# An attention, token-mixing and gating chain on one core: 512-token blocks, quarter-array attention, queries turned by VectorE, no filler matmuls

## Chip, cores and metric

The kernel runs on one core of a Trainium2 chip. The metric is the device time of one execution in microseconds; lower is better.

## What is computed

Three stages follow one another on 8 batches of 576 tokens and 512 channels. All data are 32-bit floats.

```
attn:  8 heads of 64 channels; inside chunks of 64 tokens:
       softmax(q k^T / 8) v                       -> x   (8, 576, 512)
moe:   h = relu(x^T w_tok1) w_tok2                (576 -> 256 -> 576, over tokens)
       u = x + h^T
       x2 = u + relu(u w_ch1) w_ch2               (512 -> 1536 -> 512, over channels)
moe2:  h = relu(x2 w_in); u, v = halves of h      (512 -> 2 x 512)
       v_n = layer norm of v;  v_s = w_spatial v_n + b_spatial   (over tokens)
       out = (u * v_s) w_out
```

Products with weights are made in two parts. A value is split into a high part (its fp32r rounding) and a low part (the rest), and three fp32r matmuls (high x high, high x low, low x high) add up. ScalarE makes the high part while it empties the accumulator, and VectorE makes the low part.

## The kernel before

The program is written engine by engine, with every wait given by hand as a semaphore count. The first phase makes attention and the channel mixing up to x2, batch after batch, and stores x2 in DRAM; the second phase (lines L1053 and after for TensorE) reads x2 in pairs of batches and makes the gating unit. TensorE's first phase is a list of slots.

**Channel mixing.** Each batch's 576 tokens are cut into a half of 256 and a half of 320 (`SPLIT`). For each half, 12 groups of 128 hidden channels are made by `up` (12 matmuls, L1188, into one of two `hid_bank`) and consumed by `down` (12 matmuls, L1206, into four `acc_bank`). A batch has 24 slots; slot s runs `up` of group s+2, then the side jobs of table `SIDE`, then `down` of group s. ScalarE (`hidden`, L649) and VectorE (L832) turn a finished `hid_bank` into `hidh` and `hidl`.

**Side jobs.** Between them stand the jobs that prepare the next batch: for each of its five tiles of 128 tokens (the fifth has 64) `TQ` (queries transposed by TensorE, L1106), `SC` (scores, L1115), `PT` (the probabilities transposed, L1122) and `PV` (values, L1131); then `M` (token mixing up, L1144 to L1149), and `U0`, `U1` (token mixing down plus x, L1071 to L1082) for the two halves. In `SC` a full 128x128 stationary operand with zeroed off-diagonal parts takes two heads at once. A 32-bit matmul of `SC` or `PV` appears in the trace as two instructions. Keys are turned by VectorE from the second batch on (`turn`, L788): SyncE loads them as 32-column blocks (`load_blocks`, L418, 16 DMAs of 16 KB per tile), and VectorE transposes 32x32 blocks. Queries and values come in one DMA per tile (L404).

**Order.** SyncE issues all loads and stores in program order, on one queue. `next_tiles` gives its order of the loads of the next batch. The batches 0 to 6 of the first phase are a hardware loop on every engine, as is the second phase; batch 7 is written out. The prologue (`PRO`, `PRO_ACT`, `PRO_DVE`) makes batch 0's attention and token mixing; `WARM` puts filler matmuls of the identity (L1225) ahead of some of its jobs. GpSimd clears operands, scales the probabilities in the prologue, and makes the low parts of the weights.

Of the kernel before, what the change touches and what calls it, by code (L numbers as in the profile page):

```python
# [30 lines left out]
def build(nc, q, k, v, w_tok1, w_tok2, w_ch1, w_ch2, w_in, w_spatial, b_spatial, w_out, out, x2_dram):
# [24 lines left out]
    SCALE = 1.0 / float(D) ** 0.5

    def rows(t):
        return P if t < KS else REM

    SLOTS = 2 * KF
    SIDE = {0: [("U1", 0), ("U1", 1)], 1: [("U1", 2), ("U1", 3)], 2: [("TQ", 0)], 3: [("SC", 0)], 4: [("TQ", 1)],
# [6 lines left out]

    TURN = {2: 0, 4: 1, 7: 2, 10: 3, 13: 4}

    LAST_SIDE = {0: SIDE[0], 1: SIDE[1]}
    for n in range(NT):
        LAST_SIDE[10 + n] = [("WT", n)]
    LAST_SIDE[10 + NT] = [("WR", 0), ("WR", 1)]  # L80

    def jobs(text):
        return [(kind, int(t)) for kind, t in (x.split(".") for x in text.split())]

    PRO = jobs("TQ.0 TK.0 TQ.1 TK.1 SC.0 TQ.2 TK.2 SC.1 PT.0 TQ.3 TK.3 SC.2 PV.0 PT.1 TQ.4 TK.4 SC.3 PV.1 PT.2 "
               "SC.4 PV.2 PT.3 PT.4 PV.3 PV.4 M.0 M.1 U0.0 U0.1 U0.2 U0.3")


    PRO_ACT = jobs("TQ.0 TK.0 TQ.1 TK.1 EX.0 TQ.2 TK.2 EX.1 PT.0 TQ.3 TK.3 EX.2 PV.0 PT.1 TQ.4 TK.4 EX.3 PV.1 PT.2 "
                   "TW.0 TW.1 EX.4 PV.2 PT.3 PT.4 TW.2 PV.3 PV.4 CW.0 CW.1 M.0 CW.2 M.1 CW.3 U0.0 U0.1 U0.2 U0.3")
    PRO_DVE = jobs("SH.0 NO.0 SH.1 NO.1 SH.2 NO.2 PV.0 SH.3 NO.3 PV.1 SH.4 NO.4 PV.2 PV.3 PV.4 "
                   "M.0 M.1 U0.0 U0.1 U0.2 U0.3")
# [1224 lines left out]
```

## Time and profile before

| | us |
|---|---|
| time, median of 3 runs | 1360.36 (1359.75 to 1360.47) |
| the profiled execution, its own time | 1359.22 |
| its span in the profile | 1357.4 |
| TensorE busy | 1343.2 (99%) |
| VectorE busy | 528.3 (39%) |
| ScalarE busy | 418.6 (31%) |
| GpSimd busy | 64.2 (5%) |
| DMA queue of SyncE, share of 16 engines | 20.2% |

Busy time counts each engine's instructions, overlaps once. The trace models the ends of pipelined matmuls, so durations of single matmuls overlap; the distance from start to start is what one costs in a stream. Issuing DMAs is not counted as busy, but the timeline shows each issue on SyncE with its duration.

### The profile page before, as it was taken

How to read it: one execution, taken by the hardware profiler on the slowest of the kernel's cores; microseconds unless marked ns; L12 is line 12 of the kernel's file. 1: busy time of each engine (PE TensorE's matmuls, PEld its weight loads, DVE VectorE, ACT ScalarE, POOL GpSimd, SP SyncE). 2: the span in 40 equal slices, each digit the busy share in tenths (PEclk: the TensorE clock that was granted, in tenths of full speed). 3: DMA queues.
4: the chain of work that ended last, by engine and by line, in shares of the span. 5: the costliest groups of instructions: out<-in, count | busy, mean ns of one | idle time of the engine just before them, and what ended most of it. 6: DMA issues, size and time to landing. Idle time of an engine off the chain costs nothing.

```text
span 1357.4 us, 26091 instructions
## 1 busy us (share of the span) xinstructions
PE 1343.2 (99%) x9485; PEld 1291.7 (95%) x9485; DVE 528.3 (39%) x1167; ACT 418.6 (31%) x843; POOL 64.2 (5%) x45
## 2 busy tenths in 40 slices
PE   9999999999999999999999999999999999999998
PEld 9999999999999999999999999999998998998997
DVE  3343234234224324423432342234563463463461
ACT  6532133123213312321321331123433433433332
POOL 3800000000000000000000000122000000000000
PEclk9999999999999999999999999999999999999999
DMA  9523021212302211220230210312021021021002
GB/s 251 127 53 67 21 42 42 40 38 40 66 22 44 54 26 43 55 45 25 53 67 21 42 34 1 130 47 90 1 87 55 0 76 63 0 70 70 1 1 70
DMA packets 183429, 70.57 MB, mean 52 GB/s; under 512 B 159184, under 2 KB 171088, under 8 KB 183312
## 3 DMA queue, kind: packets, MB, share of 16 engines
q1 hardware_dynamic: 183312, 68.98, 20.2%
q8 instruction: 78, 1.28, 0.4%
q14 instruction: 39, 0.32, 0.1%
HBM read 50.05 MB, written 18.87 MB: 51 GB/s over the span
## 4 chain that ended last, share of the span: by engine, by line
PE 99%; issue 1%; ACT 0%; POOL 0%; POOLq 0%
PE bank L1053 31%; PE bank L1206 23%; PE bank L1188 23%; PE bank L1131 5%; PE bank L1115 5%; PE bank L1071 4%; PE bank L1144 3%; PE bank L1106 1%; PE bank L1079 1%; PE bank L1122 1%; PE bank L1225 1%; PE bank L1149 0%; PE bank L1148 0%; PE bank L1082 0%; PE bank L1165 0%
## 5 line engine op out<-in xcount | busy, mean ns | idle before, releaser
L832 DVE SCALAR_TENSOR_TENSOR hidl<-bank,hidh 128x256 fp32r<-128x256 f32 (+1 forms) x192 | 88.0, 458 | 438.6 <-ACT hidh L649 438.6
L1206 PE MATMUL bank<-hidh,w2h 128*128 128x256 f32 (+1 forms) x768 | 237.1, 309 | 0.0
L1188 PE MATMUL bank<-uh,w1h 128*128 128x256 f32 (+1 forms) x768 | 228.3, 297 | 7.8 <-issue 7.8
L1188 PE MATMUL bank<-uh,w1l 128*128 128x256 f32 (+1 forms) x768 | 227.3, 296 | 0.0
L1188 PE MATMUL bank<-ul,w1h 128*128 128x256 f32 (+1 forms) x768 | 227.3, 296 | 0.0
L1206 PE MATMUL bank<-hidh,w2l 128*128 128x256 f32 (+1 forms) x768 | 227.1, 296 | 0.0
L1206 PE MATMUL bank<-hidl,w2h 128*128 128x256 f32 (+1 forms) x768 | 226.7, 295 | 0.0
L649 ACT ACTIVATE hidh<-bank 128x256 fp32r<-128x256 f32 (+1 forms) x192 | 78.9, 411 | 456.6 <-PE bank L1188 456.6
L1188 PEld LDWEIGHTS bank<-uh,w1h 128*128 128x128 f32 x768 | 145.8, 190 | 9.9 <-issue 9.3
L1206 PEld LDWEIGHTS bank<-hidh,w2h 128*128 128x128 f32 x768 | 145.4, 189 | 1.6
L1206 PEld LDWEIGHTS bank<-hidl,w2h 128*128 128x128 f32 x768 | 145.6, 190 | 0.5
L1188 PEld LDWEIGHTS bank<-ul,w1h 128*128 128x128 f32 x768 | 145.8, 190 | 0.0
L1188 PEld LDWEIGHTS bank<-uh,w1l 128*128 128x128 f32 x768 | 145.7, 190 | 0.0
L1206 PEld LDWEIGHTS bank<-hidh,w2l 128*128 128x128 f32 x768 | 145.2, 189 | 0.0
L1053 PE MATMUL bank<-wsh,nl 128*128 128x256 f32 (+1 forms) x256 | 75.8, 296 | 0.0
L1053 PE MATMUL bank<-wsl,nh 128*128 128x256 f32 (+1 forms) x256 | 75.7, 296 | 0.0
L1053 PE MATMUL bank<-wsh,nh 128*128 128x256 f32 (+1 forms) x256 | 75.7, 296 | 0.0
L1115 PE MATMUL bank<-k_t,q_t 128*128 128x64 f32 x576 | 68.8, 271 | 0.0
L1115 PEld LDWEIGHTS bank<-k_t,q_t 128*128 128x128 f32 x576 | 67.5, 192 | 0.1
L1053 PE MATMUL bank<-x2h,winl 128*128 128x384 f32 x192 | 64.2, 334 | 0.0
L1053 PE MATMUL bank<-x2h,winh 128*128 128x384 f32 x192 | 64.2, 334 | 0.0
L1053 PE MATMUL bank<-x2l,winh 128*128 128x384 f32 x192 | 64.2, 334 | 0.0
(158 smaller groups left out, 2356.7 us busy)
## 6 DMA issues: line engine op xcount, KB each, us to landing
x2l_raw<-x_scratch SPq DMA_DIRECT2D x32, 256.0 KB, 4.3
out<-out_tile SPq DMA_DIRECT2D x32, 256.0 KB, 2.0
qn<-in_q SPq DMA_DIRECT2D x30, 256.0 KB, 3.2
vn<-in_v SPq DMA_DIRECT2D x30, 256.0 KB, 3.9
kn<-in_k SPq DMA_DIRECT2D x448, 16.0 KB, 1.7
x_scratch<-x_half SPq DMA_DIRECT2D x8, 640.0 KB, 4.2
x_scratch<-x_half SPq DMA_DIRECT2D x8, 512.0 KB, 3.3
w1l_raw<-in_moe_w_ch SPq DMA_DIRECT2D x6, 512.0 KB, 9.1
```

Of the source, the lines that this page charges most:

```text
L649: nc.scalar.activation(hidh[:, g % 3, 0:n], hid_bank[g % 2][:, 0:n], ACT.Relu).then_inc(hid_hi, 1)
L832: return nc.vector.scalar_tensor_tensor(lo, src, 0.0, hi.bitcast(F32), op0=ALU.max, op1=ALU.subtract)
L1053: last = nc.tensor.matmul(dst, w, x, start=(n == 0), stop=(n == len(operands) - 1))
L1071: last = nc.tensor.matmul(bank[:, 0:width(h)], w, x, start=(m == 0 and e == 0), stop=(m == KT - 1 and e == 2))
L1079: nc.tensor.matmul(dst, x[:, s, cs], ident_r[:, :], is_transpose=True, start=False, stop=False)
L1106: last = nc.tensor.transpose(bank[:, g * P:g * P + n], src[:, g * P:(g + 1) * P], ident[0:n, 0:n])
L1115: last = nc.tensor.matmul(bank[:, c0:c0 + CHUNK], q_t[:, t % 2, g, a, :], k_t[:, t % 2, g, a * CHUNK:(a + 1) * CHUNK], start=True, stop=True)
L1122: last = nc.tensor.transpose(bank[0:n, g * P:(g + 1) * P], prob[:, t % 2, g, 0:n // CHUNK, :].rearrange("p a k -> p (a k)"), ident[:, :])
L1131: last = nc.tensor.matmul(bank[0:n, h * D:(h + 1) * D], p_buf(i, t)[0:n, h, 0:n], nat_tile(i, "v", t)[:, h, :], start=True, stop=True)
L1144: nc.tensor.matmul(bank[:, :], w, x, start=(e == 0), stop=False)
L1188: last = nc.tensor.matmul(hid_bank[g % 2][:, 0:width(h)], w, x, start=(c == 0 and e == 0), stop=(c == KC - 1 and e == 2))
L1206: last = nc.tensor.matmul(acc_bank[c][:, 0:n], w, x, start=(f == 0 and e == 0), stop=(f == KF - 1 and e == len(ops) - 1))
```

## The change

The first phase is written anew. The second phase keeps its computation.

- **Blocks.** The 4608 tokens of all batches are cut into 9 blocks of 512 for the channel mixing, in place of 16 halves. Block j takes the first 512-64j tokens of batch j (`UA`) behind the last 64j tokens of batch j-1 (`UB`). `up` and `down` run as `up 0, up 1, down 0, up 2, down 1, ...` (`GROUPS`), with side jobs behind single groups (`PLAN`, `REST`, `SPATIAL`). Where a boundary cuts a 128-token tile, x is added by ordinary matmuls with 64 columns of the identity.
- **Quarters.** `SC` and `PV` use 64x64 operands at the four quarters of the array: 16 matmuls of 64x64 by 64 per tile each, results in two banks.
- **Queries.** From batch 1 on `TQ` is gone. SyncE loads queries as blocks, as it does keys (16 more DMAs per tile, in place of one), and VectorE turns both (`turn`). Values come in four DMAs per tile (two for the 64-row tile).
- **Loads.** `qn`, `kn` and `vn` hold two tiles each. The next load of q and k waits until VectorE has turned the tile two before; the next load of v waits for the `PV` two before. The order is the loop `for j in range(B - 1)` below. In the prologue the first loads of batch 1 stand between the channel weights.
- **Waits and hand-overs.** `q_t`, `k_t` are single buffers; `ul` is added on GpSimd (`add_low`); x2 takes the place of `uh` and is stored in eight DMAs per block.
- **Prologue.** `WARM` is empty, `M` starts in parts (`MP`) as tiles of x are ready, VectorE scales the probabilities, two groups of channel weights (`CW_EARLY`) are rounded ahead in place of four, and the others follow `hidden` of block 0 on ScalarE.
- **Loops.** All hardware loops are written out.

```diff
--- before.py
+++ after.py
+    BW = 512
+    NB = B * S // BW
+    assert NB * BW == B * S and NB == B + 1 and S - BW == REM
...
+    def share(kind, b):
+        cut = BW - REM * b
+        return (0, cut, b, REM * b) if kind == "UA" else (cut, S, b + 1, 0)
...
+    GROUPS = [("up", 0), ("up", 1)]
+    for f in range(KF):
+        GROUPS += [("down", f)] + ([("up", f + 2)] if f + 2 < KF else [])
+    NG = len(GROUPS)
+    PLAN = {2: "SC.0", 5: "SC.1", 6: "PT.0", 7: "PV.0", 8: "SC.2", 9: "PT.1", 10: "PV.1", 11: "SC.3", 12: "PT.2",
+            13: "PV.2", 14: "SC.4", 15: "PT.3", 16: "PV.3", 17: "PT.4", 18: "PV.4", 19: "M.0", 20: "M.1",
+            21: "UA.0 UA.1", 22: "UA.2 UA.3"}
+    REST = {3: "UB.0 UB.1", 4: "UB.2 UB.3"}
+    SPATIAL = {9: "WT.0", 10: "WT.1", 11: "WT.2", 12: "WT.3", 13: "WT.4", 14: "WR.0", 15: "WR.1"}
+    def behind(j, g):
+        if j > B - 1:
+            return []
+        side = jobs(j, REST.get(g, ""))
+        if j < B - 1:
+            return side + jobs(j + 1, PLAN.get(g, ""))
+        return side + jobs(0, SPATIAL.get(g, ""))
+    PRO_PE = jobs(0, "TQ.0 TK.0 TQ.1 TK.1 SC.0 TQ.2 TK.2 SC.1 PT.0 TQ.3 TK.3 PV.0 SC.2 PT.1 TQ.4 TK.4 PV.1 SC.3 PT.2 "
+                     "PV.2 SC.4 PT.3 MP.0 PV.3 PT.4 MP.1 PV.4 MP.2 MP.3 M.0 M.1 UA.0 UA.1 UA.2 UA.3")
+    PRO = [job for job in PRO_PE if job[0] != "MP"]
+    PRO_ACT = jobs(0, "TQ.0 TK.0 TQ.1 TK.1 EX.0 TQ.2 TK.2 EX.1 PT.0 TQ.3 TK.3 EX.2 PV.0 PT.1 TQ.4 TK.4 EX.3 PV.1 PT.2 "
+                      "TW.0 TW.1 EX.4 PV.2 PT.3 TW.2 PV.3 PT.4 CW.0 PV.4 CW.1 M.0 M.1 UA.0 UA.1 UA.2 UA.3")
+    PRO_DVE = jobs(0, "SH.0 NO.0 SH.1 NO.1 SH.2 NO.2 PV.0 SH.3 NO.3 PV.1 SH.4 NO.4 PV.2 PV.3 PV.4 "
+                      "M.0 M.1 UA.0 UA.1 UA.2 UA.3")
...
-    WARM = {("TQ", 0): 9, ("TQ", 1): 6, ("TQ", 2): 8, ("PV", 2): 7, ("PT", 4): 2}
+    WARM = {}
...
+            def load_v(b, t):
+                for h2 in range(2):
+                    for a in range(rows(t) // CHUNK):
+                        s0 = t * P + a * CHUNK
+                        src = v_in[b, :, s0:s0 + CHUNK, :].rearrange("(g e) s d -> e s g d", e=2)
+                        sp.dma_start(v_tile(b, t)[h2 * CHUNK:(h2 + 1) * CHUNK, :, a, :],
+                                     src[h2, :, :, :]).then_inc((v_loaded if b > 0 else v_first)[t], DMA)
+            def load_blocks(buf, src, b, t, loaded):
                 for h2 in range(2):
                     for e in range(D // BLK):
                         p0 = h2 * D + e * BLK
-                        dst = k_blocks(t)[p0:p0 + BLK, :].rearrange("p (g j e) -> p g j e", g=PAIRS, e=BLK)
+                        dst = blocks(buf, b, t)[p0:p0 + BLK, :].rearrange("p (g j e) -> p g j e", g=PAIRS, e=BLK)
                         for g in range(PAIRS):
-                            src = k[b, 2 * g + h2, t * P:t * P + rows(t), e * BLK:(e + 1) * BLK]
+                            part = src[b, 2 * g + h2, t * P:t * P + rows(t), e * BLK:(e + 1) * BLK]
                             sp.dma_start(dst[:, g, :, :],
-                                         src.rearrange("(j r) e -> r j e", r=BLK)).then_inc(k_loaded[t], DMA)
-            for t in range(NT + 2):
+                                         part.rearrange("(j r) e -> r j e", r=BLK)).then_inc(loaded[t], DMA)
+            def load_qk(b, t):
+                n = later(b, t)
+                if n >= 2:
+                    sp.wait_ge(q_t_ready, NT + n - 1)
+                    sp.wait_ge(k_t_ready, NT + n - 1)
+                load_blocks(qn, q_in, b, t, q_loaded)
+                load_blocks(kn, k_in, b, t, k_loaded)
+            def load_v_next(b, t):
+                n = later(b, t)
+                if n >= 2:
+                    sp.wait_ge(side_full, number["PV", 1 + (n - 2) // NT, (n - 2) % NT])
+                load_v(b, t)
+            for t in range(NT + 1):
                 if t < NT:
...
+                if g == 1:
+                    load_qk(1, 0)
+                if g == 2:
+                    load_v_next(1, 0)
+                    load_qk(1, 1)
+                if g == 3:
+                    load_v_next(1, 1)
...
+            for j in range(B - 1):
+                b = j + 1
+                if j > 0:
+                    store_x2(j - 1)
+                more = b + 1 < B
+                load_qk(b, 3)
+                load_qk(b, 4)
+                load_v_next(b, 2)
+                if more:
+                    load_qk(b + 1, 0)
+                load_v_next(b, 3)
+                if more:
+                    load_qk(b + 1, 1)
+                load_v_next(b, 4)
+                if more:
+                    load_qk(b + 1, 2)
+                    load_v_next(b + 1, 0)
+                    load_v_next(b + 1, 1)
...
+            def add_low(j):
+                for c in range(KC):
+                    pool.wait_ge(acc_free, KC * j + c + 1)
+                    nc.gpsimd.tensor_tensor(x2[j % 2][:, c, :], x2[j % 2][:, c, :], ul[j % 2][:, c, :].bitcast(F32),
+                                            ALU.add).then_inc(x2_ready, 1)
...
+                        if j == 0 and f < NCW - CW_EARLY:
+                            channel_high(CW_EARLY + f)
...
+            def turn(b, t):
+                n = tile_no(b, t)
+                loads = b * (4 * PAIRS * DMA)
+                before = (b, t - 1) if t > 0 else (b - 1, KS)
+                dve.wait_ge(side_full, number[("SC",) + before])
+                for buf, dst, loaded, ready in ((qn, q_t, q_loaded, q_t_ready), (kn, k_t, k_loaded, k_t_ready)):
+                    dve.wait_ge(loaded[t], loads)
+                    nc.vector.transpose(dst[:, :, 0:rows(t)].bitcast(U32),
+                                        blocks(buf, b, t).bitcast(U32).rearrange("p (g s) -> p g s", g=PAIRS)
+                                        ).then_inc(ready, 1)
...
+                    two, qt, kt = both(job), q_tile(b, t), k_tile(b, t)
                     for g in range(PAIRS):
-                        for a in range(2 if t < KS else 1):
-                            c0 = (2 * g + a) * CHUNK
-                            last = nc.tensor.matmul(bank[:, c0:c0 + CHUNK], q_t[:, t % 2, g, a, :],
-                                                    k_t[:, t % 2, g, a * CHUNK:(a + 1) * CHUNK], start=True, stop=True)
+                        for e in range(2):
+                            for a in range(n // CHUNK):
+                                r, s = slice(e * D, (e + 1) * D), slice(a * CHUNK, (a + 1) * CHUNK)
+                                last = nc.tensor.matmul(two[s, e, g * CHUNK:(g + 1) * CHUNK], qt[r, g, s], kt[r, g, s],
+                                                        start=True, stop=True)
...
+                    two, pt, vt = both(job), p_tile(b, t), v_tile(b, t)
+                    for g in range(PAIRS):
+                        for e in range(2):
+                            for a in range(n // CHUNK):
+                                r, s = slice(e * CHUNK, (e + 1) * CHUNK), slice(a * CHUNK, (a + 1) * CHUNK)
+                                last = nc.tensor.matmul(two[s, e, 256 + g * D:256 + (g + 1) * D], pt[r, g, s],
+                                                        vt[r, g, a, :], start=True, stop=True)
...
+            for job in PRO_PE:
+                kind, _, t = job
+                for _ in range(WARM.get((kind, t), 0)):
+                    nc.tensor.matmul(hid[:, 1, 0:P], ident[:, :], ident[:, :], start=True, stop=True)
+                if kind == "MP":
+                    pe.wait_ge(part_lo, parts["PV", 0, t])
+                    if t == 0:
+                        pe.wait_ge(wlo, 2)
+                    for m in range(KT):
+                        token_up(m, hid[:, m, :], t)
+                else:
+                    side_job(job)
+
```

## Rows read from the trace of the kernel before

**Rows 1.** The page, its part 4: shares of the chain that ended last.

```profile
PE 99%; issue 1%; ACT 0%; POOL 0%; POOLq 0%
```

**Rows 2.** Windows by stage: prologue, five whole batches, second phase (columns in first line).

```profile
core 0: us, PE busy (x) PEld busy (x) DVE busy (x) ACT busy (x) POOL busy (x), PEclk, DMA share, GB/s
0.00:45.74 45.74, 43.26 (x344) 41.05 (x345) 16.39 (x33) 32.55 (x54) 24.28 (x22) 1.00 1.01 250
...
164.33:741.27 576.94, 570.27 (x4400) 560.27 (x4401) 209.32 (x421) 153.45 (x315) 0.00 (x0) 1.00 0.20 43
...
937.81:1357.40 419.59, 415.65 (x2336) 381.44 (x2336) 195.13 (x497) 148.75 (x302) 0.00 (x0) 1.00 0.13 43
```

**Rows 3.** Waits of TensorE: in total, times, longest.

```profile
PE bank L1188 <- issue: 7.8, 6, 1.5
```

**Rows 4.** Timeline of SyncE: start, us, k blocks of the last batch, 16 issues each.

```profile
755.67 7.47 SPq L418 DMA_DIRECT2D kn<-in_k  x16
...
765.40 8.30 SPq L418 DMA_DIRECT2D kn<-in_k  x16
...
776.71 8.63 SPq L418 DMA_DIRECT2D kn<-in_k  x16
```

**Rows 5.** The page, its part 6: KB each, median us to landing.

```profile
vn<-in_v SPq DMA_DIRECT2D x30, 256.0 KB, 3.9
kn<-in_k SPq DMA_DIRECT2D x448, 16.0 KB, 1.7
```

**Rows 6.** Timeline of TensorE: first and last of 512, 256 and 320 column runs.

```profile
35.65 0.39 PE L1144 MATMUL bank<-xh,t1h 128*128 128x512 f32 x1
...
37.47 0.39 PE L1144 MATMUL bank<-xh,t1l 128*128 128x512 f32 x1
...
53.74 0.28 PE L1206 MATMUL bank<-hidh,w2h 128*128 128x256 f32 x1
...
54.70 0.28 PE L1206 MATMUL bank<-hidh,w2l 128*128 128x256 f32 x1
...
699.75 0.31 PE L1188 MATMUL bank<-uh,w1h 128*128 128x320 f32 x1
...
701.37 0.31 PE L1188 MATMUL bank<-uh,w1l 128*128 128x320 f32 x1
```

**Rows 7.** Timeline of TensorE: a TQ, a PV of 64 rows, an SC, with neighbours.

```profile
61.86 0.60 PE L1106 MATMUL bank<-ident,qn 128*128 128x128 f32 x4
...
62.22 0.36 PE L1206 MATMUL bank<-hidh,w2h 128*128 128x256 f32 x1
...
128.68 0.31 PE L1188 MATMUL bank<-uh,w1l 128*128 128x320 f32 x1
128.92 1.14 PE L1131 MATMUL bank<-vn,p_t 64*64 64x64 f32 x16
...
130.24 0.31 PE L1206 MATMUL bank<-hidl,w2h 128*128 128x320 f32 x1
...
650.23 1.90 PE L1115 MATMUL bank<-k_t,q_t 128*128 128x64 f32 x16
651.93 0.36 PE L1206 MATMUL bank<-hidh,w2h 128*128 128x256 f32 x1
```

**Rows 8.** Groups by line and form, VectorE: busy us, mean ns, idle before.

```profile
L801 DVE TENSOR_REDUCE smax<-bank 128x8 f32<-128x512 f32 x32 | 22.1, 692 | 45.9 <-PE bank L1115 45.8
...
L788 DVE STREAM_TRANSPOSE k_t<-kn 128x512 uint32<-128x512 uint32 x28 | 19.7, 702 | 0.0
```

**Rows 9.** Timeline of SyncE in the prologue.

```profile
17.18 0.77 SPq L427 DMA_DIRECT2D t1l_raw<-in_moe_w_tok  x1
...
19.82 0.47 SPq L434 DMA_DIRECT2D w1l_raw<-in_moe_w_ch  x1
```

**Rows 10.** Timeline of TensorE: the first and the fourth group of filler matmuls.

```profile
1.53 3.94 PE L1225 MATMUL bank<-ident 128*128 128x128 f32 x18 [1.53 <-POOL ident L539]
...
26.15 1.78 PE L1225 MATMUL bank<-ident 128*128 128x128 f32 x14
```

More of the change, by code:

```diff
@@ L103, in listing @@
-    def listing(table):
-        return [j for s in range(SLOTS) for j in table.get(s, [])]
-    BODY, LAST = listing(SIDE), listing(LAST_SIDE)
-    PRO_BANKS = 6
-    def order(i):
-        return PRO if i is None else (LAST if isinstance(i, int) and i == B - 1 else BODY)
-    def bank_of(i, idx):
-        return idx % (PRO_BANKS if i is None else 2)
-    def number(i, job):
-        return order(i).index(job) + 1
-    def parts(i, job):
-        seq = order(i)
-        return sum(j[0] in TWO_PART for j in seq[:seq.index(job) + 1])
@@ L129, in build, with tile_no @@
+    number = {job: n + 1 for n, job in enumerate(SEQ)}
+    parts = {}
+    for job in SEQ:
+        if job[0] in TWO_PART:
+            parts[job] = len(parts) + 1
+    in_bank = {n: [job for job in SEQ if n in BANKS[job]] for n in range(8)}
+    def tile_no(b, t):
+        return b * NT + t
     with ExitStack() as ctx:
@@ L277, in build @@
         side_full = sem("side_full")
-        side_free = [sem(f"side_free{b}") for b in range(PRO_BANKS)]
         q_t_ready = sem("q_t_ready")
@@ L518, in store_out @@
                                      out_tile[bb * REM:(bb + 1) * REM, n % 2, :]).then_inc(s, DMA)
-            def pair(j, last):
-                if not last:
+            for j in range(NP):
+                if j < NP - 1:
                     sp.wait_ge(full, j * NJ + job_no(("U", NU - 1)))
@@ L567, in _ @@
                 split(c, winh[:, c, :], winl_raw[:, c, :], winl[:, c, :])
+            add_low(B - 1)
+            add_low(NB - 1)
             pool.wait_ge(wout_loaded, DMA)
+            for c in range(KC):
+                pool.wait_ge(x2_stored[c], stored(NB - 1))
             for c in range(KC):
@@ new lines, in _ @@
+            for j in range(NB):
+                if j > 0:
+                    residual(j - 1)
+                for g, (kind, f) in enumerate(GROUPS):
+                    if kind == "up":
+                        hidden(j, f)
+                    if j == 0 and g == 1:
+                        turn(1, 0)
+                    for job in behind(j, g - 1) if g > 0 else []:
+                        if job[0] == "SC":
+                            softmax_norm(job[1], job[2])
+                    for job in behind(j, g):
+                        if job[0] == "SC":
+                            softmax_shift(job[1], job[2])
+                            n = later(job[1], job[2]) + 1
+                            if n < (B - 1) * NT:
+                                turn(1 + n // NT, n % NT)
+                        elif job[0] in TWO_PART:
+                            side_job(job)
@@ L937, in stats @@
+            for piece in range(KC):
+                split_x2(0, piece)
+            residual(NB - 1)
+            for b in range(4, 8):
+                dve.sem_inc(free[b], 1)
+            for piece in range(KC, X2_PIECES):
+                split_x2(0, piece)
             def stats(j, n):
@@ L1008, in gate_low @@
                 r.then_inc(g_lo, 1)
-            def pair(j, last):
-                gates = [m for kind, m in PHASE2 if kind == "SP"]
+            dve.wait_ge(bias_loaded, DMA)
+            for j in range(NP):
                 for n in range(NJ):
@@ L1085, in side, with token_up @@
[L1085 to L1104 removed]
+            def token_up(t, bank, s):
+                cols = slice(t * P, (t + 1) * P)
+                for e, (w, x) in enumerate(three(t1h[:, s, cols], t1l[:, s, cols], xh[:, s, :], xl[:, s, :])):
+                    nc.tensor.matmul(bank, w, x, start=(s == 0 and e == 0), stop=False)
```

828 lines of the change are left out of this document (353 added, 475 removed), and 6 rows, old and new, of the table SIDE.

## The prediction

> **What bounds the kernel now.** I read the page first: the chain that ended last is TensorE for 99% [rows 1]. TensorE's waits come next: 7.8 us in six stops of up to 1.5 us, released by no engine; they stand where the batch loop turns [rows 3]. So before, time is the sum of TensorE's instructions. The windows cut it: 45.74 us of prologue, 576.94 us for five batches (115.4 each), 419.59 us of second phase [rows 2], which the change leaves alone. Then the queue that the change loads most: SyncE, where the k blocks of the batch written out without a loop show what one DMA issue costs [rows 4].
>
> **TensorE, part by part.** Pitches from start to start: 512 columns (37.47 - 35.65)/8 = 0.227 us; 256 columns 0.96/8 = 0.120; 320 columns 1.62/11 = 0.147 [rows 6]. Each is the columns at 2.4 GHz plus 0.013.
> - `up` and `down`: before 8 x 24 x 12 = 2304 matmuls at 0.120 and as many at 0.147, 615 us. After 9 x 24 x 12 = 2592 at 0.227, 588 us. Gain 27.
> - Loop turns gone: gain 8 [rows 3].
> - `TQ` gone in 7 batches: a job costs 0.36 us plus 0.08 on the next matmul [rows 7], so some 0.44 x 28 plus 7 of the short tile, 15 us.
> - `SC` and `PV` in quarters. A full-array `SC` takes 1.70 us for 16 instructions, 0.107 each. The only quarter jobs in the trace are the `PV` of the 64-row tile: 16 instructions, and from 128.68 to 130.24 they cost 1.56 - 2 x 0.147 = 1.27 us; 1.14 busy less a matmul's tail is about 0.93, or 0.058 each, and 0.34 is for going into and out of that shape [rows 7]. After, a tile has 32 such instructions. One at a time: 32 x 0.058 + 0.34 = 2.2 us. Four at a time: 0.46 + 0.34 = 0.8. No row shows two quarters side by side. I take 1.5, the middle, since 2.2 is the nearest row but all its instructions used the same quarter. Over 56 jobs that is a gain of 56 x (1.78 - 1.5) = 16 (1.78: the 1.70 and 0.08 on the next matmul), between a loss of 24 and a gain of 55.
> - Token mixing: same columns; 32 extra matmuls where tiles are cut and a few narrow ones: loss 4, bounds 2 and 6.
>
> The row says that a lone 64-row job pays 0.34 us for its shape and that its instructions follow at 0.058. The Trainium skill (TensorEngine Tiling (Array Packing), Key Properties) has a rule for each side: changing the tiling mode drains the engine, and different tiles execute weight loads and matmuls in parallel. By the first alone the 56 jobs would lose 24 us; with both they would gain 55.
>
> TensorE's own work after the prologue would then be: 588 + 84 (56 x 1.5) + 15 (14 short `SC` and `PV` at 1.1) + 16 (`PT`) + 45 (`M`, 14 jobs of 14 matmuls at 0.227) + 74 (token mixing) + 3 (the spatial transposes) = 825 us, against 892 (937.81 - 45.74) before.
>
> **VectorE, ScalarE, GpSimd.** A turn costs VectorE 0.70 us, twice per tile now, in place of once [rows 8]; per block about 5 x 0.7 us more on an engine 39% busy. ScalarE loses the two `TQ` copies. GpSimd gets `add_low`, free after the prologue. I cost these at nothing as long as `turn` finds its data; but `turn` waits for a DMA inside VectorE's queue, and behind it stand the low parts that `down` waits for.
>
> **SyncE: the new chain.** Before, a tile took 16 DMAs for k, one for q, one for v. After, 32 for q and k, and 4 for v: 178 per batch in place of 90. Three straight runs of 16 took 7.47, 8.30 and 8.63 us [rows 4], so one issue costs 24.4/48 = 0.508 us (0.467 to 0.539). It is the queue's pace, not the transfer: a block lands 1.7 us after issue [rows 5]. A tile's q and k need 32 x 0.508 = 16.3 us, while `SC` jobs stand three groups apart: 3 x 12 x 0.227 = 8.2 us plus some 2 of side jobs. Only two tiles of buffer stand between.
>
> Follow block j (1 to 5), from its start. `SC.0` stands behind group 2: 8.2 + 1.7; then the two VectorE passes over the scores and the two turns of tile 1, 4 x 0.7 = 2.8, and 0.3 for semaphores: 13.0. Only now may SyncE load tile 3. Its order up to the values of tile 4 is q,k 3; q,k 4; v 2; q,k 0 of the next batch; v 3; q,k 1 of the next batch; v 4. That is 128 + 10 = 138 issues x 0.508 = 70.1, plus 2 to land: 85.1. TensorE would want `PV.4` at about 74 (19 groups x 2.72 = 51.7 plus the side jobs before it, 22), so it stops some 11 us. Behind `PV.4` (1.3) come five groups (13.6), `M` (6.4) and `UA` (4.0 on average): 25.3. A block takes 110.4 us, whatever the quarters cost; five take 552.
>
> Block 0 is later still, since SyncE comes to it from the prologue. The first channel weight was issued at 19.82 [rows 9]; 13 more v issues push it to between 20 and 26, I take 23. From there to the last value of tile 4 of batch 1 stand 12 weight DMAs, 7 tiles of q and k (224) and 18 of v: 254 x 0.508 = 129.0. So 23 + 129 + 2 = 154, and with the tail (`PV.4` 1.3, groups 13.6, `M` 6.4, `UA` of 448 columns 6.4) block 0 ends at 181.7. The prologue itself hides: its first `up` I put at 49 (45.74 plus 3 for the 256 columns that move into it), and its missing fillers cost nothing on this chain. ScalarE's wait for the fourth weight group inside block 0 hides behind it too.
>
> Block 6 has no next loads in front of its values and is TensorE's own: 65.4 + 12 + 2.2 + 2.3 + 6.4 + 9 = 97. Block 7 is 65.4 + 8.5 + 3 = 77, block 8 is 65.4.
>
> **Sum.** 181.7 + 552 + 97 + 77 + 65.4 = 973.1; 1 for the hand-over; 419.6 for the second phase: span 1393.7.
>
> The stops also cost clock. Each stretch of the trace reads a granted clock of 1.00 [rows 2], yet the first group of fillers, after 1.53 us of idle, took 3.94/18 = 0.219 us per instruction and a later one 1.78/14 = 0.127 [rows 10]: the 1.2 GHz level against the 2.4 GHz level, 18 x 0.092 = 1.7 us lost. Six stops at `PV.4` of some 10 us: 10.2 (bounds 0 and 15). Span 1404; 1.8 around it (1359.22 against 1357.4) and 1.1 up to the median (1360.36 against 1359.22): **1407 us**.
>
> The bounds: at 0.467 per issue the chain's 254 + 690 issues take 39 less, and without clock loss 10 less: 1358. At 0.539 they take 29 more, and the prologue 3: 1439. Quarters at 2.2 add about 11 (`SC.0` and `PV.4` in six blocks, all jobs in block 6).
>
> **Rivals.**
> - *SyncE keeps up (faster).* Mechanism: the issue pace in straight code is set by something that the new program doesn't have, and each q,k tile is there when `turn` asks. For it: SyncE needs only 186 issues per block, stores among them, 94 of 110 us, so it isn't full, only badly placed; DMA engines are 20% busy. Against it: 0.47 stands between nearly all issues of the three runs. Then TensorE's sum holds: 49 + 825 + 419.6 + 3 + 3 = 1300 us (quarters between: 1258 to 1341). It decides below about 0.46 us per issue: the chain must lose 47 us over 944 issues, 0.05 each, for the forecast to meet 1360.
> - *Half of it.* The chain exists, but stops hide in block slack, and gains and stops cancel: about 1360.
> - *Code fetch and queue.* All code is straight now. The runs of rows 4 differ by single slow issues (7.47 against 8.63 for the same 16). If such gaps grow with the doubled list, one issue costs 0.56 and the chain gives 1407 + 944 x 0.052 = 1456.
> - *Quarters one at a time*: 1418, within the forecast's range.
>
> The Trainium skill (DMA: Bandwidth & Descriptors, Anatomy of one DMA, written for the other descriptor path) gives about 50 ns for the dispatch of a DMA and says that many descriptors can be emitted before their cost shows. By that price the 944 issues would take 47 us and the first rival would hold; the rows of SyncE show ten times as much, and the measurement decides.
>
> **Chances.** Forecast (1358 to 1439): 0.60. SyncE keeps up: 0.31. Half: 0.04. Code fetch: 0.05. So faster by over 0.2%: 0.32; within 0.2%, about what a measurement of this kernel can tell from no change: 0.04; slower: 0.64. The range reaches down to 1295, which leaves out about four tenths of the first rival, and up to 1440: together 0.2 left out. The forecast's own range is 1358 to 1439.
>
> **What would show it.** In the profile after: SyncE's q and k issues back to back for most of a block, 16 in about 8 us; TensorE idle ahead of `PV` of the last tile, released by a DMA of v, some 10 us in each of blocks 0 to 5, and in block 0 stops ahead of several jobs; first phase's blocks of 110 us, then 97, 77 and 65. VectorE's turns with idle time released by DMA of q. `up` and `down` at 0.227. The quarters show as distances within `SC` and `PV`: 0.058 is one at a time. The prediction is wrong if issues of q and k come faster than 0.46 us, if TensorE has no stops, or if the second phase is longer than 420 us.

## The result

The changed kernel takes 1416.05 us (median of 4 runs, 1415.86 to 1417.48) against 1360.15 for the one before: a ratio of 1.0413, 95% interval [1.0395, 1.0431]. It is slower by 56 us. The profiled execution's span is 1414.0 us.

The page of the changed kernel, its parts 1, 2 and 4. TensorE is busy for fewer microseconds than before (1289.0 in place of 1343.2), and the chain that ended last, all TensorE before [rows 1], is now SyncE's queue for a quarter:

```profile
PE 1289.0 (91%) x8385; PEld 1091.8 (77%) x8385; DVE 527.7 (37%) x1079; ACT 335.7 (24%) x647; POOL 102.2 (7%) x73
...
PEclk8897799799889889979979999999999999999999
...
PE 69%; SPq 26%; issue 3%; DMA 1%; DVE 0%; ACT 0%
SPq L459 22%; PE hid L1147 15%; PE acc L1162 14%; PE acc L1027 13%; PE hid L1027 8%; PE side L1027 8%; SPq L449 3%; PE side L1036 3%; PE side L1062 2%; PE side L1048 2%; DMA vn<-in_v 1%; PE side L1055 1%; PE side L1105 1%; PE side L1089 1%; SPq L441 1%
```

L459 issues the blocks of q and k, L449 the values. `up` is L1147, `down` L1162, `SC` L1089, `PT` L1094, `PV` L1105. The waits of TensorE (us in total, times, longest) name above all one transfer; the stops of [rows 3] are gone:

```profile
PE side L1105 <- DMA vn<-in_v: 97.2, 14, 9.1
PE side L1078 <- DMA q_pro<-in_q: 5.3, 2, 4.3
PE acc L1078 <- DVE xl L832: 3.9, 1, 3.9
```

Windows of the changed kernel, cut at the first `up` (57.44), at the starts of blocks 1 and 6 (192.20, 757.70) and at the end of block 8 (994.53), with the columns of [rows 2]:

```profile
0.00:57.44 57.44, 40.56 (x432) 31.42 (x433) 22.17 (x40) 24.26 (x41) 15.74 (x13) 0.82 0.64 157
57.44:192.20 134.76, 107.38 (x710) 86.46 (x708) 42.62 (x73) 27.76 (x46) 19.90 (x9) 0.85 0.28 59
192.20:757.70 565.50, 488.69 (x3542) 397.75 (x3540) 197.61 (x356) 99.18 (x185) 25.54 (x21) 0.91 0.21 42
757.70:994.53 236.83, 236.83 (x1371) 194.76 (x1369) 69.87 (x119) 45.02 (x83) 28.48 (x21) 1.00 0.17 50
994.53:1414.00 419.47, 415.55 (x2337) 381.38 (x2335) 195.48 (x494) 139.45 (x293) 12.55 (x12) 1.00 0.13 43
```

Where SyncE has loads of the next batch ahead of its values (blocks 0 to 5), TensorE idles and its granted clock is below 1. Blocks 6 to 8 and the second phase have no idle time beyond the usual, and the clock is 1.00. The second phase is that of before (419.59). So the whole loss stands in the prologue and in blocks 0 to 5.

SyncE's timeline in block 2 (306.16 to 421.51): start, time over which the issues run, count.

```profile
317.87 9.06 SPq L459 DMA_DIRECT2D qn<-in_q  x16
326.98 7.55 SPq L459 DMA_DIRECT2D kn<-in_k  x16
334.62 8.24 SPq L459 DMA_DIRECT2D qn<-in_q  x16
...
363.27 7.67 SPq L459 DMA_DIRECT2D kn<-in_k  x16
370.99 2.58 SPq L449 DMA_DIRECT2D vn<-in_v  x4
373.66 7.66 SPq L459 DMA_DIRECT2D qn<-in_q  x16
381.37 7.55 SPq L459 DMA_DIRECT2D kn<-in_k  x16
388.96 1.26 SPq L449 DMA_DIRECT2D vn<-in_v  x2
```

And TensorE's in the same block, its two long stops and what follows the first (a third stop, of 1.4 us, stands ahead of `PV.2`):

```profile
375.87 1.13 PE L1105 MATMUL side<-vn,p_t 64*64 64x64 f32 x32 [9.09 <-DMA vn<-in_v]
376.93 0.79 PE L1147 MATMUL hid<-uh_a,w1h 128*128 128x512 f32 x1
...
377.94 0.63 PE L1147 MATMUL hid<-uh_a,w1l 128*128 128x512 f32 x1
378.37 0.63 PE L1147 MATMUL hid<-uh_a,w1h 128*128 128x512 f32 x1
...
392.18 1.12 PE L1105 MATMUL side<-vn,p_t 64*64 64x64 f32 x16 [6.85 <-DMA vn<-in_v]
```

From 317.87 to 390.22 SyncE issues without a break (the three rows left out are of the same kinds). The four value DMAs of tile 3 end at 373.57 and land 2.3 us later: there `PV.3` starts. The two of tile 4 end at 390.22 and land 2.0 us later: there `PV.4` starts. Behind the stop a 512-column matmul takes 0.43 us (378.37 - 377.94) in place of 0.227.

### The profile page after: what moved, and what is told of

Same layout as the page of the kernel before. It is cut to its first block, busy times and chain, and to the rows that moved or that the text cites. A ratio compares the mean times of both kernels' runs of the same rounds, so it can differ in the third digit from the quotient of the medians.

```text
span 1414.0 us, 20802 instructions
## 1 busy us (share of the span) xinstructions
PE 1289.0 (91%) x8385; PEld 1091.8 (77%) x8385; DVE 527.7 (37%) x1079; ACT 335.7 (24%) x647; POOL 102.2 (7%) x73
## 2 busy tenths in 40 slices
DMA packets 226495, 70.35 MB, mean 50 GB/s; under 512 B 203296, under 2 KB 213152, under 8 KB 226400
## 3 DMA queue, kind: packets, MB, share of 16 engines
q1 hardware_dynamic: 226400, 69.02, 20.0%
## 4 chain that ended last, share of the span: by engine, by line
PE 69%; SPq 26%; issue 3%; DMA 1%; DVE 0%; ACT 0%
SPq L459 22%; PE hid L1147 15%; PE acc L1162 14%; PE acc L1027 13%; PE hid L1027 8%; PE side L1027 8%; SPq L449 3%; PE side L1036 3%; PE side L1062 2%; PE side L1048 2%; DMA vn<-in_v 1%; PE side L1055 1%; PE side L1105 1%; PE side L1089 1%; SPq L441 1%
## 5 line engine op out<-in xcount | busy, mean ns | idle before, releaser
L1162 PE MATMUL acc<-hidh,w2h 128*128 128x512 f32 x432 | 176.5, 409 | 0.0
L1162 PE MATMUL acc<-hidl,w2h 128*128 128x512 f32 x432 | 170.3, 394 | 0.0
L1162 PE MATMUL acc<-hidh,w2l 128*128 128x512 f32 x432 | 170.2, 394 | 0.0
L1105 PE MATMUL side<-vn,p_t 64*64 64x64 f32 x1008 | 29.9, 254 | 97.2 <-DMA vn<-in_v 97.2
L1105 PEld LDWEIGHTS side<-vn,p_t 64*64 64x64 f32 x1008 | 24.9, 161 | 110.1 <-issue 110.1
L1147 PE MATMUL hid<-uh_a,w1h 128*128 128x512 f32 x240 | 103.6, 432 | 0.0
L1147 PE MATMUL hid<-ul_a,w1h 128*128 128x512 f32 x240 | 99.4, 414 | 0.0
L1147 PE MATMUL hid<-uh_a,w1l 128*128 128x512 f32 x240 | 98.7, 411 | 0.0
L1162 PEld LDWEIGHTS acc<-hidh,w2l 128*128 128x128 f32 x432 | 82.1, 190 | 18.2
L1162 PEld LDWEIGHTS acc<-hidh,w2h 128*128 128x128 f32 x432 | 82.1, 190 | 17.6
L1162 PEld LDWEIGHTS acc<-hidl,w2h 128*128 128x128 f32 x432 | 82.3, 190 | 15.1
L1147 PE MATMUL hid<-uh_b,w1h 128*128 128x512 f32 x192 | 82.8, 431 | 0.0
L1147 PE MATMUL hid<-ul_b,w1h 128*128 128x512 f32 x192 | 79.3, 413 | 0.0
L1147 PE MATMUL hid<-uh_b,w1l 128*128 128x512 f32 x192 | 78.8, 410 | 0.0
L1147 PEld LDWEIGHTS hid<-uh_a,w1h 128*128 128x128 f32 x240 | 48.7, 203 | 11.4
L1147 PEld LDWEIGHTS hid<-uh_a,w1l 128*128 128x128 f32 x240 | 48.5, 202 | 11.2
L665 ACT ACTIVATE prob<-prob 128x512 f32<-128x512 f32 (+1 forms) x40 | 25.3, 632 | 130.6 <-DVE prob L815 130.6
L1147 PEld LDWEIGHTS hid<-ul_a,w1h 128*128 128x128 f32 x240 | 48.9, 204 | 9.4
```

The costliest lines, as they stand in the source:

```text
L1105: last = nc.tensor.matmul(two[s, e, 256 + g * D:256 + (g + 1) * D], pt[r, g, s], vt[r, g, a, :], start=True, stop=True)
L1147: last = nc.tensor.matmul(hid[:, n % 2, :], w, x, start=(c == 0 and e == 0), stop=(c == KC - 1 and e == 2))
L1162: last = nc.tensor.matmul(acc[:, c, :], w, x, start=(f == 0 and e == 0), stop=(f == KF - 1 and e == len(ops) - 1))
```

## The experiments

Times are medians, ratios are to the kernel before as run beside each. The main theory: SyncE issues a DMA every 0.5 us, the loads of q, k stand ahead of the values in one queue, and their number sets the length of a block. The rivals were the quarters, the filler matmuls, and the turning of queries as such.

### Queries in one DMA per tile

```diff
-                load_blocks(qn, q_in, b, t, q_loaded)
+                sp.dma_start(qn[0:rows(t), n % 2, :].rearrange("p (h d) -> p h d", h=H),
+                             q_in[b, :, t * P:t * P + rows(t), :].rearrange("h s d -> s h d")).then_inc(q_loaded[t], DMA)
...
```

> The changed kernel, but from batch 1 on a tile's queries come in one DMA in place of 16, in their natural layout, and VectorE turns that; what is left out is the right layout of q, so scores of batches 1 to 7 are of other numbers, while every instruction on TensorE, VectorE and ScalarE stays. SyncE issues 103 DMAs per batch in place of 178. Theory (the issues of SyncE set the blocks): the 97 us of TensorE stops ahead of PV go, and the first phase falls to TensorE's own sum, 57 (prologue) + 795 + 419.5 = 1272 us of span, 1275 measured. Rival (the stops come from something else, such as the values' four DMAs, code written out without loops, or VectorE's second transpose): above 1380.

1278.77 us, ratio 0.9406 [0.9387, 0.9425], span 1276.7, near the theory's 1275. No wait for values is left; the largest of TensorE's are now those of the prologue:

```profile
PE side L1079 <- DMA q_pro<-in_q: 5.4, 3, 4.2
PE acc L1106 <- DVE xl L833: 4.9, 2, 3.7
```

Blocks 1 to 5 run from 156.62 to 620.38, TensorE busy in every microsecond:

```profile
156.62:620.38 463.76, 463.76 (x3541) 378.84 (x3540) 197.06 (x356) 99.19 (x185) 25.54 (x21) 1.00 0.23 51
```

This run gives the split of the loss. For the same instructions the changed kernel took 565.50 us: 76.8 of idle time and 488.69 - 463.76 = 24.9 of slower matmuls. The idle time is ten stops of 6.7 to 9.1 us and the one of 1.4, so that a long stop is 7.5 us of waiting and some 2.5 us of slow clock. Fifteen issues fewer per tile bring 137 us in all. The bytes are the same (the same tile in one piece). The packets fall too, from 226,400 to 185,744 on this queue, but the 16 engines were busy for 20.0% with them and are for 21.0% without, and a block of 16 KB landed 1.8 us after its issue. So what costs is the number of issues, not the transfers.

### The value loads on another queue

ScalarE issues the values of the tile two later once it has emptied a `PV`; SyncE keeps all loads of q and k.

```diff
-                if n >= 2:
-                    sp.wait_ge(side_full, number["PV", 1 + (n - 2) // NT, (n - 2) % NT])
-                load_v(b, t)
+                if n < 2:
+                    load_v(b, t)
...
+                    m = later(b, t) + 2
+                    if b > 0 and m < (B - 1) * NT:
...
+                                act.dma_start(v_tile(vb, vt)[h2 * CHUNK:(h2 + 1) * CHUNK, :, a, :],
+                                              src[h2, :, :, :]).then_inc(v_loaded[vt], DMA)
```

> The changed kernel, but the values of batches 1 to 7 (from their third tile) are issued by ScalarE right after it has emptied the PV of two tiles before, in place of SyncE behind 64 to 128 issues of q and k. Same DMAs, same data, other queue. Theory: the values no longer stand behind q and k, the stops ahead of PV go; what is left is the pace of q and k, seen as VectorE waiting in turn for k of the next batch: blocks 1 to 5 of 97 to 101 us in place of 113, total about 1330 (1310 to 1350). Rival (issue pace is shared by all queues, or the transfer itself is slow): 1390 or more.

1329.28 us, ratio 0.9777 [0.9758, 0.9797], as the theory had it (1330). The wait for values is gone; what is late next is one step up the same queue. Waits of TensorE, and of VectorE for a DMA:

```profile
PE side L1102 <- DVE xl L840: 23.5, 6, 5.3
...
DVE k_t L811 <- DMA kn<-in_k: 67.2, 12, 8.8
```

VectorE stands in `turn`, waiting for k, with the low part of x queued behind (L840), and TensorE's next `PT` (L1102) waits for the bank that VectorE has yet to read. So 87 us of the changed kernel's loss come from the values standing behind q and k on one queue (118 value issues have also left SyncE), and some 50 stay with the number of q and k DMAs (1329 against 1279).

### Values ahead of the next batch's q and k, same queue

```diff
                 load_v_next(b, 2)
-                if more:
-                    load_qk(b + 1, 0)
                 load_v_next(b, 3)
                 if more:
-                    load_qk(b + 1, 1)
+                    load_qk(b + 1, 0)
                 load_v_next(b, 4)
                 if more:
+                    load_qk(b + 1, 1)
                     load_qk(b + 1, 2)
```

> The changed kernel with SyncE's order alone changed: v of tile 3 ahead of q and k of the next batch's tile 0, v of tile 4 ahead of its tile 1. The same number of issues. Theory (what counts is how many issues stand in front of the last values): 34 fewer issues ahead of v of tile 4; the stop moves to VectorE, whose turn waits for the next batch's tile 0, and with it to PT.4; blocks of about 102 us in place of 113, total 1350 (1335 to 1375). Rival (SyncE is simply full, and order doesn't matter): 1416 within 5.

1350.52 us, ratio 0.9934 [0.9914, 0.9954]. Not a DMA more or fewer, 66 us less, as the theory had it (1350): order alone turns the change from a loss into a gain of 0.7%. The waits move as before, to VectorE behind `turn`:

```profile
PE side L1093 <- DVE xl L831: 39.4, 6, 8.6
PE side L1104 <- DMA vn<-in_v: 9.4, 2, 8.5
```

### The filler matmuls back

```diff
-    WARM = {}
+    WARM = {("TQ", 0): 9, ("TQ", 1): 6, ("TQ", 2): 8, ("PV", 2): 7}
```

> The changed kernel with filler matmuls back ahead of TQ.0, TQ.1, TQ.2 and PV.2 of the prologue (9, 6, 8 and 7; the two ahead of PT.4 stay out, since their bank is in use now). Theory (SyncE's list sets where block 0 ends): the first up starts earlier, by 5 to 9 us, and block 0 ends where it did, because its end hangs on the 254 issues after the first channel weight: total within 3 us of 1416. Rival (the prologue's loss of 11.7 us, 57.4 against 45.7, is on the path): 1404 to 1410.

1414.84 us, ratio 1.0404 [1.0386, 1.0421]: within the interval of the changed kernel. Leaving the fillers out costs nothing here that can be measured. The total is what the theory said, but not by its way: its first `up` stands at 56.30 in place of 57.45, 1.2 us earlier and not 5 to 9. So the fillers save little in this prologue even before SyncE's chain can hide it; the runs further down come back to this.

### Queries turned by TensorE again

As the first experiment, but with the whole computation: one natural DMA per tile of q, and `TQ` jobs in the plan.

```diff
-    PLAN = {2: "SC.0", 5: "SC.1", 6: "PT.0", 7: "PV.0", 8: "SC.2", 9: "PT.1", 10: "PV.1", 11: "SC.3", 12: "PT.2",
-            13: "PV.2", 14: "SC.4", 15: "PT.3", 16: "PV.3", 17: "PT.4", 18: "PV.4", 19: "M.0", 20: "M.1",
+    PLAN = {1: "TQ.0", 2: "SC.0", 4: "TQ.1", 5: "SC.1", 6: "PT.0 TQ.2", 7: "PV.0", 8: "SC.2", 9: "PT.1 TQ.3",
+            10: "PV.1", 11: "SC.3", 12: "PT.2 TQ.4", 13: "PV.2", 14: "SC.4", 15: "PT.3", 16: "PV.3", 17: "PT.4", 18: "PV.4", 19: "M.0", 20: "M.1",
...
-                for buf, dst, loaded, ready in ((qn, q_t, q_loaded, q_t_ready), (kn, k_t, k_loaded, k_t_ready)):
+                for buf, dst, loaded, ready in ((kn, k_t, k_loaded, k_t_ready),):
...
```

> The whole computation, with queries of batches 1 to 7 turned by TensorE again: one natural DMA per tile, TQ jobs in the slots 1, 4, 6, 9 and 12 of the plan. SyncE then has 16 issues fewer per tile and VectorE one transpose fewer. Working from the run with queries in one DMA (1278.8 us): 28 full TQ jobs at 0.46 and 7 short ones at 0.62 us are 17 us of TensorE. Theory (the queue was the bound of the change, and turning queries by VectorE was the edit that cost, not the one that paid): 1279 + 17 = 1296, between 1285 and 1302, and no wait on values. Rival (turning queries by TensorE brings waits on ScalarE's emptying back at five places per batch, 0.5 us each or more): above 1302.

1363.19 us, ratio 1.0033 [1.0021, 1.0045]. The time lies where the rival put it, but both theories missed the reason: there is no wait on values, the `TQ` jobs run at their price (0.45 us), and the waits ahead of `TQ.0` are 6.5 us in all, but seven stops of 6 us stand ahead of `UB` (L1049). TensorE's and ScalarE's waits:

```profile
PE side L1049 <- DVE ul_b L833: 22.7, 4, 7.8
PE side L1049 <- DVE ul_a L833: 20.1, 3, 7.3
...
ACT uh_a L654 <- DMA x_scratch<-x_a: 33.4, 6, 10.8
ACT uh_b L654 <- DMA x_scratch<-x_b: 33.0, 6, 11.1
```

Timelines around one of them: SyncE's, then TensorE's `TQ.0` (L1083), then ScalarE's hand-over of `UB` (L654):

```profile
229.45 2.53 SPq L449 DMA_DIRECT2D vn<-in_v  x2
271.08 0.39 SPq L468 DMA_DIRECT2D qn<-in_q  x1
271.52 8.84 SPq L459 DMA_DIRECT2D kn<-in_k  x16
280.40 5.22 SPq L449 DMA_DIRECT2D vn<-in_v  x8
285.67 0.60 SPq L509 DMA_DIRECT2D x_scratch<-x_b  x1
```

```profile
269.79 0.60 PE L1083 MATMUL side<-ident,qn 128*128 128x128 f32 x4
```

```profile
288.46 0.32 ACT L654 CAST uh_b<-side 128x192 fp32r<-128x192 f32 x1 [11.10 <-DMA x_scratch<-x_b]
```

SyncE's load of tile 2 of the next batch waits until `TQ.0` has freed its buffer. In the changed kernel `turn` of tile 0 frees it inside the block before, and that load follows the last value at once (390.32 behind 390.22). `TQ.0` runs in the next block (269.79), so SyncE stood from 231.98 to 271.08, and the stores of x2, next in its order, left at 285.67, though the block had started at 264.34; in the changed kernel they leave 0.5 us after the start (306.66 against 306.16). `uh_b` takes over the space that they read. A wait whose release I had moved from the end of one block into the next held the whole queue.

### The stores ahead of the loads that wait

```diff
                 more = b + 1 < B
+                if j > 0:
+                    load_v_next(b, 0)
+                    load_v_next(b, 1)
+                    load_qk(b, 2)
                 load_qk(b, 3)
...
-                if more:
-                    load_qk(b + 1, 2)
-                    load_v_next(b + 1, 0)
-                    load_v_next(b + 1, 1)
```

> The kernel with queries turned by TensorE (1363.2 us), with one change of the order on SyncE: the loads of tile 2 and the value loads of tiles 0 and 1 of the next batch go behind the stores of x2, in place of ahead of them. In the profile of that kernel SyncE stood from 232 to 271 us waiting for TQ.0, which runs one block later, with the stores of x2 queued behind; ScalarE's uh_b and uh_a waited for these stores (66.4 us), and TensorE for VectorE's ul behind ScalarE (42.8 us). Theory (a wait for a TQ of the next block held the queue, and the held stores were the whole loss): these waits of TensorE go, and some 15 to 20 us of slow clock with them (granted clock 0.969 against 0.992): 1296, between 1288 and 1304. Rival (TQ on TensorE costs more than its jobs' time, wherever the stores stand): above 1315.

1300.86 us (1300.36 to 1302.18), ratio 0.9566 [0.955, 0.9582], within the theory's range. All 42.8 us of waits ahead of `UB` but 2.8 are gone, TensorE is busy for 98%, and this kernel, which computes everything, is faster than the one before and the changed one. Queries turned by TensorE cost 1300.9 - 1278.8 = 22 us over the first experiment, in which q does not get its right layout: 17 of jobs as worked out, and 6.5 of waits for the hand-over of `UB` ahead of `TQ.0`:

```profile
PE side L1083 <- DVE ul_b L833: 3.7, 4, 1.3
PE side L1083 <- DVE ul_a L833: 2.8, 3, 1.2
```

### Fillers where TensorE sets the end

The same line of `WARM`, in the two kernels with `TQ` on TensorE.

> As the kernel with queries turned by TensorE, with 9, 6, 8 and 7 filler matmuls back ahead of TQ.0, TQ.1, TQ.2 and PV.2 of the prologue. In the changed kernel they were worth only 1.2 us, within its interval, because SyncE's chain of loads set the end of block 5. Here TensorE sets it, so that what the fillers save in the prologue stays: before, the same jobs ran at a TQ price of 0.60 to 0.66 in place of 1.09 us there and the first up came at 45.7 in place of 57.4 us. Theory: 3 to 10 us faster than without them, about 1289. Rival (the slow clock of the prologue has another cause, its own matmuls being too few): within 1.5 us of the kernel without them.

1362.89 us (1357.86 to 1367.04) against 1363.19 without them: these runs spread too widely to show 3 us.

> As the kernel with the stores first, with 9, 6, 8 and 7 filler matmuls ahead of TQ.0, TQ.1, TQ.2 and PV.2 of the prologue. Where the stores were held they were worth 0.3 us, within its interval. Theory (the held queue hid them): 3 to 10 us faster than the same kernel without them, about 1290. Rival (the fillers save nothing in this prologue, whose own waits set its end): within 1.5 us of it.

1301.09 us (1299.57 to 1302.33) against 1300.86. My theory fell twice, and the second time nothing hid them. With fillers the first `up` stands at 55.27, without at 54.35. The windows from 20 to 45 us, without fillers and with them:

```profile
20.00:45.00 25.00, 15.60 (x208) 12.14 (x208) 11.70 (x23) 14.02 (x23) 10.96 (x6) 0.86 0.72 214
```

```profile
20.00:45.00 25.00, 17.99 (x222) 14.76 (x222) 11.42 (x22) 13.41 (x22) 10.10 (x5) 0.80 0.68 201
```

TensorE is busy for 18 of 25 us with the fillers. The granted clock doesn't settle what they do: it is 0.80 here against 0.86 without, but 0.83 against 0.59 in the same window of the changed kernel, whose prologue is the same. Stops settle the time. Two without fillers, and the start of `M` (L1037) with them:

```profile
23.26 0.46 PE L1083 MATMUL acc<-ident,q_pro 64*128 64x64 f32 x4 [4.03 <-DVE xl L833]
...
30.59 1.00 PE L1110 MATMUL acc<-v_pro,p_t 64*64 64x64 f32 x32 [3.68 <-DVE xl L833]
```

```profile
35.11 0.47 PE L1037 MATMUL hid<-xh,t1h 128*128 128x512 f32 x1 [2.13 <-POOL t1rem_l L596]
```

The fillers shorten the second of the two stops to 1.41 us, and then TensorE waits 2.13 us ahead of `M` for the low part of the token weights, which GpSimd finishes at 34.96. Without them the same part is finished at 33.54 and `M` starts at 33.68, and in the changed kernel at 34.94 and 35.09: in all of these runs `M` stands right behind its weights. So what the fillers save ahead of `M` is lost in front of it.

The first stop is hardly VectorE's extra work, as I first thought. VectorE now scales the probabilities in the prologue, which GpSimd did before, but its order is the same list, and in the kernel before it made the first `xl` at 21.99, less than a microsecond earlier than here (22.52). There `TQ.4` had run at 20.61, ahead of it. What has changed is the bank: before, the jobs of the prologue went round six banks one by one; now they go round three pairs (`BANKS`), and `TQ.4` gets the pair of `PV.0`, which is free only behind that `xl`. No run changed the banks or gave the scaling back to GpSimd, so this is read from the traces and not tested.

### Four matmuls in a row on one quarter

On the kernel with `TQ` on TensorE (1363.19): the loops of `SC` and `PV` change places, so that four matmuls in a row use the same quarter.

```diff
-                    for g in range(PAIRS):
-                        for e in range(2):
-                            for a in range(n // CHUNK):
+                    for e in range(2):
+                        for a in range(n // CHUNK):
+                            for g in range(PAIRS):
```

> The kernel with queries turned by TensorE, in which the 16 matmuls of a score or value job are ordered so that four follow one another on the same quarter of the array, in place of going round the four quarters. Same matmuls, same banks, same waits. Theory (a quarter matmul is cheap only because the next goes to another quarter, and on the same quarter it waits out its own 64 columns, about 0.05 us an instruction as bounded by the pitch of the 64-column rows of before): a 32-instruction job costs about 1.6 to 2.2 in place of 0.84 us, 72 of them with 16 short ones 60 to 110 us more. Rival (the order makes no difference, a quarter matmul is cheap by itself): within 4 us of the kernel without the new order, a job at 0.84 us.

1422.8 us, ratio 1.0467 [1.0446, 1.0487]: 60 us more, at the lower edge of the theory (which counted 72 jobs of 32 instructions; there are 64). A job with its neighbours, in turn around the quarters (changed kernel), and four in a row (this one):

```profile
337.41 0.39 PE L1162 MATMUL acc<-hidh,w2l 128*128 128x512 f32 x1
337.73 0.69 PE L1089 MATMUL side<-k_t,q_t 64*64 64x64 f32 x32
338.35 0.50 PE L1147 MATMUL hid<-uh_a,w1h 128*128 128x512 f32 x1
338.69 0.39 PE L1147 MATMUL hid<-ul_a,w1h 128*128 128x512 f32 x1
```

```profile
244.02 0.39 PE L1152 MATMUL hid<-uh_b,w1l 128*128 128x512 f32 x1
244.34 1.54 PE L1110 MATMUL side<-vn,p_t 64*64 64x64 f32 x32
245.81 0.51 PE L1167 MATMUL acc<-hidh,w2h 128*128 128x512 f32 x1
246.15 0.40 PE L1167 MATMUL acc<-hidl,w2h 128*128 128x512 f32 x1
```

From the matmul before to the second after: 1.28 us less two of 0.227 is 0.83 us for 32 instructions in turn; 2.13 less 0.45 is 1.68 us in a row. Over all jobs between such matmuls the medians are 0.83 and 1.67, and for those of 16 instructions 0.81 and 1.09. The differences add up to the whole: 64 x 0.84 + 16 x 0.28 = 58 of the 60 us. So a quarter is cheap because the next instruction goes to another quarter.

The four numbers also give an estimate of a job's parts. In a row an instruction costs (1.67 - 1.09)/16 = 0.036 us and the rest of a job 1.67 - 32 x 0.036 = 0.52. In turn a quarter gets eight instructions in either job: the one of 32 uses four quarters, the one of 16 two. 0.52 + 8 x 0.036 = 0.81, which is what both take, as if the quarters ran fully side by side.

The Trainium skill (TensorEngine Tiling (Array Packing), Key Properties) says that different tiles can load weights and multiply in parallel, and these two orders agree. Its other rule is that changing the tiling mode drains the engine. From the last wide matmul to the first quarter one it is 0.32 us (337.73 - 337.41), where it is 0.24 to a `PT` job, which keeps the whole array (330.62 to 330.86): this agrees, and puts the entry at some 0.08 us.

## Why the prediction came out near

Predicted 1407, measured 1416. The mechanism is the one forecast, and the first experiments show it by taking it away. Term by term:

- *SyncE's price of an issue: right.* 0.508 was taken; in the changed kernel a distance within q and k is 0.474 at the median and 0.505 in the mean (1050 of them). The rival in which SyncE keeps up needed less than 0.46.
- *The chain of a block: right.* 13.0 + 70.1 + 2 + 25.3 = 110.4, plus 1.7 for clock, against 113.1 (565.50/5). The four parts, as means of blocks 1 to 5: SyncE is released 11.8 us after the block's start, the 138 issues take 71.3, the last value lands 2.0 later, and the tail behind it is 28.1. The tail was taken 2.8 short; the slow clock behind the stop, which I had counted apart, is in it.
- *Where it shows: half right.* One stop of 11 us ahead of `PV.4` was forecast. There are two, of 7 to 9 us, ahead of `PV.3` and of `PV.4`, some 15 together (and one of 1.4 us ahead of `PV.2` in block 2). Both wait for the queue. TensorE asked for `PV.4` earlier than assumed, since the quarters are cheaper than I had them; the chain's length doesn't depend on it.
- *Block 0: right in kind, 10 us short.* The first channel weight left at 25.24 (23 taken), the 254 issues took 133.6 (129.0 taken, 0.526 each in place of 0.508), the last value landed 2.4 later, and `PV.4` to the block's end took 30.9 (161.32 to 192.20) in place of 27.7.
- *Quarters: mis-sized.* 1.5 us per job taken, between 0.8 and 2.2; 0.83 measured. I chose the middle because the only row showed a single quarter; the bound for four at a time was the true one, and by luck in its parts: 0.46 + 0.34 were taken, some 0.29 + 0.52 are what the runs give. On the SyncE chain the jobs cost nothing, and so the error didn't reach the total. On TensorE's sum it is 56 x 0.67 + 14 x 0.29 = 42 us too much. That sum (825) came out at about 801: 1276.7 - 56.2 - 419.5 in the first experiment. Against the 42 stand token mixing, 82 us by the distances where 74 was taken, and 3 us of a wait; some 7 us I can't place.
- *Blocks 6 to 8: near.* 97, 77 and 65.4 were said; 93.9, 77.7 and 65.3 measured. In block 6 the quarters were taken 6 us too high, so that the rest of it was some 3 too low.
- *The prologue: first `up` at 49 forecast, 57.4 measured.* The step that failed is "45.74 plus 3". The wider `UA` costs 4.0 (49.00 to 57.45 in place of 41.33 to 45.74), near the 3. The other 7.7 come before it, and almost all of them after `M` starts, which it does at 35.09 as it did before (34.87): 3.0 us are the last `PV` and `PT` jobs, which now stand between the parts of `M`; 2.9 are `M`'s own matmuls, 12 of which take 0.43 us; 1.6 go on waiting for `ml`. "45.74 plus 3" left the prologue's jobs in their old time and their old order, and put new waits at nothing. The stops of 3.9 and 3.7 us for `xl` further ahead look like the reason why cheaper attention jobs did not bring these `PV` in front of `M`. The forecast that the prologue hides behind SyncE's chain held: the chain of block 0 starts at the weight issues, not at the first `up`.
- *The clock: mechanism right, price low.* 1.7 us per stop taken from [rows 10], six stops; 2.5 us measured, ten long stops in blocks 1 to 5 alone: 24.9 us, and 10.1 more in block 0 (107.38 busy against 97.30 in the first experiment). The bounds of 0 and 15 were too narrow. It reached the total only in part: what is slow between two stops of a block ends in the second stop, which waits for SyncE all the same.
- *The total.* Without clock the sum was a span of 1393.7; measured 1414.0. Block 0 is 10.5 us longer, blocks 1 to 5 are 13.5, block 6 is 3 shorter, the end 1. The 10.2 added for clock cover half of it.
- *The rival in which SyncE keeps up* is the first experiment: 1300 was worked out for it, 1279 measured: 24 less from TensorE's sum, 7 more from the prologue, and 4 less in the small terms at the end. Its condition, an issue below 0.46, isn't met with the q blocks in.
- *Half* and *quarters one at a time* fell: no cancelling in the blocks, and 0.83 us per job.
- *Code fetch:* 0.56 per issue was its condition; 0.505 was measured in straight code, over a list of 1442 issues.

The Trainium skill (DMA: Bandwidth & Descriptors, Anatomy of one DMA) gives about 50 ns for the dispatch step of a DMA on GpSimd's path. Here an issue on SyncE lasted ten times that, as in the rows of before; for a queue of many small DMAs the measured distance is the price.

So the change holds a gain of 59 us (1360.3 against 1300.9), which blocks of 512, quarters and straight loops bring together and no run takes apart, and one edit, the loads of q in blocks, that costs 115 by its place and number against the whole kernel without it (1416.0 against 1300.9). What stays open is what the prologue would gain from other banks, from earlier weights for `M`, or from GpSimd's scaling.

## What to carry to other kernels

Count the instructions of each DMA queue, times its measured pace, as one counts TensorE's columns: a queue whose 16 engines are 20% busy can still be what sets the time. Then read its order as a chain: what waits in it, what stands behind that wait, and who waits for those; the same DMAs in another order were worth 66 us here, and a wait whose release moved into the next block, with the stores behind it, cost 62 (1363.2 against 1300.9). And before an engine's work is moved to save its time, price what the other form asks of the queues.

## What was new about the hardware

- Quarter-array matmuls of 64x64 by 64 in turn around the quarters: a job of 32 instructions on four quarters costs 0.83 us and one of 16 on two quarters 0.81. In a row on one quarter 32 cost 1.67 and 16 cost 1.09, which is 0.036 us each and some 0.52 for the rest of the job.
- A DMA's issue on SyncE takes as long for 16 KB (0.47 to 0.57 us each in runs of 16) as for a natural tile of 256 KB of q (0.37 to 0.61 in the first experiment), and 0.65 for 64 KB of values (2.59/4); what sets a queue's time is how many it issues.
- After 7 to 9 us of idle time TensorE goes on at the 1.2 GHz level (0.43 us for 512 columns in place of 0.227); such a stop costs some 2.5 us beyond itself (24.9 us for ten).
